# Moving ScalarE's splits of weight chunks 2 and 3 behind the decayed keys and the increments of the first group

## The reference

```python
for t in range(S):          # S = 768, B = 2, H = 8 heads, D = 48
    cur = einsum('bhd,bhe->bhde', u[None] * kt, vt)
    y[:, :, t] = einsum('bhd,bhde->bhe', rt, state + cur)
    state = wt[:, :, :, None] * state + einsum('bhd,bhe->bhde', kt, vt)
x = y as 1536 rows of 384
x = (maximum(x @ w_in, 0) ** 2) @ w_out              # d_ff = 2048
logits = x @ w_gate; each row goes to the best of 8 experts (1024 wide),
out[i] = gate_w[i] * (maximum(x[i] @ w1[e], 0) @ w2[e])
```

## Time and profile before

| what | value |
|---|---|
| device time, median of 3 runs | 469.6 us (468.51 to 470.47) |
| the profiled execution's own time | 469.28 us |
| its span | 467.6 us |
| PE busy, share of the span | 437.4 us (94%) |
| DVE busy | 313.5 us (67%) |
| ACT busy | 252.1 us (54%) |

### The profile page before, as it was taken

One profiled execution on the slowest core, in us unless ns is written; L12 is line 12 of the kernel. 1 busy time (PEld: TensorE's weight loads), 2 busy tenths in 40 slices (PEclk: granted clock), 3 DMA queues, 4 the chain that ended last, 5 costly groups with the idle time before them and its releaser, 6 DMA issues.

```text
span 467.6 us, 15105 instructions
## 1 busy us (share of the span) xinstructions
PE 437.4 (94%) x6263; PEld 415.4 (89%) x6263; DVE 313.5 (67%) x786; ACT 252.1 (54%) x515; POOL 52.3 (11%) x64
## 2 busy tenths in 40 slices
PE   3769999999999999999999999999999789999993
PEld 3658999999999999999999999988998679999993
DVE  4978866757786768677867737657547976688410
ACT  1153875356535654565455566564548875686420
POOL 6000000000000100001000100221021333421201
PEclk9999999999999999999999999999999999999998
DMA  7726795790140014001000157522776998420000
GB/s 262 254 79 197 274 322 181 255 354 4 45 146 1 3 48 178 1 3 38 3 1 4 37 209 265 162 93 70 278 236 192 341 330 272 153 59 1 30 17 27
DMA packets 35644, 63.44 MB, mean 136 GB/s; under 512 B 3980, under 2 KB 21950, under 8 KB 35568
## 3 DMA queue, kind: packets, MB, share of 16 engines
q1 hardware_dynamic: 33264, 57.88, 36.4%
q0 software_dynamic: 2304, 4.47, 2.6%
HBM read 50.77 MB, written 14.19 MB: 139 GB/s over the span
## 4 chain that ended last, share of the span: by engine, by line
PE 78%; DVE 9%; DMA 4%; issue 4%; ACT 3%; SPq 1%; POOL 0%; DVEq 0%; POOLq 0%; ACTq 0%
PE bank L683 21%; PE bank L669 19%; PE bank L885 5%; PE pair L588 5%; PE bank L838 4%; PE pair L550 3%; DMA stage<-in_moe_w_in 3%; PE pair L853 3%; PE bank L853 3%; PE bank L892 3%; PE pair L838 3%; DVE KRW L1153 2%; PE pair L609 2%; ACT W L924 2%; DVE AD L1172 2%
## 5 line engine op out<-in xcount | busy, mean ns | idle before, releaser
L669 PE MATMUL bank<-XH,W 128*128 128x256 f32 x576 | 119.0, 283 | 0.0
L683 PE MATMUL bank<-W,GH 128*128 128x384 f32 x372 | 98.9, 347 | 0.0
L669 PEld LDWEIGHTS bank<-XH,W 128*128 128x128 f32 x576 | 94.6, 188 | 0.7
L669 PE MATMUL bank<-XL,W 128*128 128x256 f32 x288 | 80.5, 280 | 0.0
L1018 ACT ACTIVATE RB<-bank 128x256 f32<-128x256 f32 x96 | 36.8, 383 | 55.6 <-PE bank L669 55.0
L683 PEld LDWEIGHTS bank<-W,GH 128*128 128x128 f32 x372 | 62.0, 188 | 1.3
L683 PE MATMUL bank<-W,GL 128*128 128x384 f32 x186 | 62.7, 337 | 0.0
L1209 DVE TENSOR_TENSOR GL<-GG,GH 128x256 fp32r<-128x256 f32 x96 | 40.5, 422 | 29.5 <-ACT GH L924 29.0
L924 ACT ACTIVATE GH<-GG 128x256 fp32r<-128x256 f32 x96 | 40.3, 420 | 35.9 <-PE bank L683 34.0
L588 PE MATMUL pair<-KRW 48*64 48x32 f32 (+1 forms) x2304 | 46.2, 228 | 11.9 <-DMA KRW<-in_krw 6.5
L588 PEld LDWEIGHTS pair<-KRW 48*64 48x64 f32 (+1 forms) x2304 | 40.4, 143 | 18.7 <-DVE KRW L1154 7.0
(11 more groups left out here) (162 smaller groups left out, 695.3 us busy)
## 6 DMA issues: line engine op xcount, KB each, us to landing
raw<-in_moe_w SPq DMA_DIRECT2D x23, 768.0 KB, 8.5
stage<-in_moe_w SPq DMA_DIRECT2D x9, 768.0 KB, 9.2
KRW<-in_krw SPq DMA_DIRECT2D x12, 512.0 KB, 6.3
slots<-X SPq DMA_DIRECT2D x8, 579.0 KB, 5.6
VV<-in_v SPq DMA_DIRECT2D x12, 288.0 KB, 6.9
KRW<-in_krw SPq DMA_DIRECT2D x12, 256.0 KB, 6.5
stage<-in_moe_w_in SPq DMA_DIRECT2D x4, 768.0 KB, 7.3
stage<-in_moe_w_out SPq DMA_DIRECT2D x4, 768.0 KB, 7.0
```

The costliest lines, as they stand in the source:

```text
L669: last = nc.tensor.matmul(bank[4 + f % 2][:, 0:2 * P], win[wa][:, c, f * P:(f + 1) * P], xa[:, c, :], start=n == 0, stop=n == 3 * KM - 1)
L683: last = nc.tensor.matmul(bank[6 + m][:, 0:DM], ga[(NF * g + f) % G3][:, cols], wout[wa][:, f, :], start=f == 0 and n == 0, stop=f == NF - ...
```

## The change

One row of numbers is edited:

```diff
-    HIGH_SLOT = (0, 1, 4, 6, 17, 19, 21, 23)
+    HIGH_SLOT = (0, 1, 6, 8, 17, 19, 21, 23)
```

## The result

| kernel | median | runs | mean | profiled execution |
|---|---|---|---|---|
| before | 471.29 us | 20 | 471.10 | 469.28 (span 467.6, mean granted clock 0.997) |
| the change | 468.44 us (465.74 to 470.46) | 20 | 468.63 | 468.20 (span 466.2, clock 0.988) |

The ratio is 0.995 (95% interval 0.9934 to 0.9966): 1.6 to 3.1 us faster. The three runs of the kernel before that the forecast started from had a median of 469.6. Twenty runs put it at 471.29. The change's median of 468.44 lies above the forecast range, which ended at 468.0, though it is faster, as forecast.

The account below looks back on a forecast made before the run. The prediction took the ramp, where ACT's list holds attention for chunk 2's load, as what can be won, PE bounding the rest. x_low ending 37.93 - 34.85 = 3.1 us earlier gave 466.2 to 466.5, forecast 466.3; 8-in-10 range 465.2 to 468.0.

Parts of the forecast that it names:

- The mechanism: First group's ramp: ACT's in-order list holds the attention for chunk 2's load; moving the split removes PE's 3.00 us pause.
- 469.28 - 3.1 = 466.2: Whole kernel: the profiled execution's time less the ramp's gain, which should stand unchanged at the end.
- DVE is the later by 0.3 us: End of the first group: DVE's weighted keys end at 33.61, XH of tile 0 is there at 33.35.
- the unread ones end at about 31.2: PE's nine unread matmuls between the tiles' state outputs end then, so tile 1's start at 31.66, 3.3 us earlier.
- 2.33 us behind: PE, first group: the unread matmuls end the same distance as before behind tile 0's state outputs.
- the fast sum: Ramp with PE at the fast pace: x_low ends at 34.85 instead of 37.93, 3.1 us gained.
- The fast pace: PE's transposes and products after the removed pause: run at 2.4 GHz, as PE was taken to run before it.
- The slow sum: Ramp with PE at the slow pace: XH decides the end, 3.0 us gained.
- instead of 27.10: 3.0 us earlier: PE's first transposes (kk_rows) start at about 24.1, no longer held by chunk 2's landing and split.
- The pause was ACT's doing: Rival: something else holds the transposes, so the time stays 469.3, no change; chance 0.05.
- Chunk 4 kept its advance: Rival: chunk 4's load loses one to two microseconds of its advance, 467.2 to 468.4; partial losses, loads or pace, 0.14.
- The slow pace did not stay on: Rival: PE stays slow from increments to the multilayer stage, 468.2 or slower; partial losses, loads or pace, 0.14, slower 0.03.

Follow-up runs that it names:

- chunk3_only: Only chunk 3's split moved behind the increments, chunk 2's left ahead of the level copies as in the kernel before; ratio 1.0008 to the kernel before.
- before_early2: The kernel before with SP's load of chunk 2 issued ahead of the second group's first tile, ACT's order unchanged; median 468.5 us, ratio 0.9941.
- warm_levels: The change plus one unread TensorE matmul ahead of each tile's levels 3, 4 and 5 in the first group; one execution, 471.81 us.
- low2_late: The change with DVE's low part of chunk 2 moved behind x_low (slot 12); one execution, 470.85 us.
- change_again: The changed kernel run once more, unaltered; median 468.43 us, ratio 0.9951 to the kernel before.
- chunk2_at5: The change with chunk 2's split right behind the level copies, ahead of the decayed keys' copies; one execution, 471.26 us.
- no_unread9: The change without the nine unread TensorE matmuls between the two tiles' state outputs; one execution, 474.55 us, where the kernel before took 473.58.
- the five traces with a cover: Kernels before or changed, one also with chunk 2 loaded early, with nine unread matmuls added at the changeover, three of them with six more; medians 468.0 to 471.19 us.
- the six extra matmuls: Six more unread matmuls ahead of the wait for expert 3's weights, added to three kernels with a cover; medians 471.19, 468.51 and 469.17 us.
- before_cover: The kernel before with nine unread TensorE matmuls, three at each of three waits for VectorE at the changeover; median 470.69 us, ratio 0.9994.

## Why the prediction came out as it did

**The mechanism held.** The level copies moved to right behind level 5, the transposes lost their 3.0 us of idle time, no wait for a chunk appeared, the state's chain followed the low parts, and chunk 3 between IN and KRW cost nothing. chunk3_only showed that chunk 2's move is the whole gain, before_early2 that it is the wait for the landing.

**The gain was 2.4 us, not 3.1, and the base was 1.8 us too low.** "469.28 - 3.1 = 466.2" failed in three terms, here from the smallest to the largest.

**PE's side of the ramp, 0.2 us.** The sum's 3.1 us was 2.89 between the two profiled ramps. The step that failed is "DVE is the later by 0.3 us" at the end of the group. DVE's own part was right: 10.0 us from its first low part to the end of x_low, as in warm_levels. But XH was the later by 0.28 us, and low2_late showed that PE decides. Behind it is "the unread ones end at about 31.2", 6.35 us behind the start of DVE's low parts. They ended 7.30 us behind it in the trace after. The slow pace of the transposes and products isn't the whole reason. In change_again the increments were fast and tile 0's IN was there 3.9 us behind the start of the low parts instead of 4.6, yet the unread matmuls ended 7.29 us behind it and the stretch was 10.17:

```profile
25.01 1.60 PE L609 MATMUL pair<-VV,AD 64*64 64x48 f32 x64
26.44 1.10 PE L621 MATMUL pair<-VV,UK 64*64 64x48 f32 x64
27.70 0.67 PE L644 MATMUL pair<-IN,KRW 48*64 48x48 f32 x16 [0.15 <-ACT IN L924]
29.23 1.84 PE L657 MATMUL bank<-W 128*128 128x384 f32 x9 [0.86 <-issue]
```

The 0.86 us are idle time for which the profile names no wait. Before had 0.48 at the same place, which the prediction carried along in its "2.33 us behind". In twelve traces (all but chunk2_at5 and no_unread9) the unread matmuls start 6.07 to 6.46 us behind the first transpose, whether the increments took 1.10 or 1.92 us. What sets that distance is open. So the fast sum failed by its link from IN to the unread matmuls, and a faster pace alone would not have made it true.

The fast pace itself was a misreading of the earlier trace rows. I took 32 matmuls of level 5 in 0.66 us for the fast pace. Those load 32 columns of weights instead of 64. By form in before's trace, ahead of the pause and in the second group:

```profile
L588 PE MATMUL pair<-KRW 48*32 48x32 f32 x32 | 0.7, 240 | 0.6 <-DVE KRW L1154 0.6
```

```profile
L588 PE MATMUL pair<-KRW 48*32 48x32 f32 x64 | 0.8, 196 | 0.0
```

240 ns for one against 196: PE had been slow before the pause too, so the pause had cost no pace. The Trainium skill ("TensorE: Matmul & The Clock Gate", Part 1) was applied to a fast state that did not exist here. Its two levels agree with the granted clocks of 0.50 and 1.00 in no_unread9 and with two durations of a transpose, 423 and 273 ns, and its throttled default agrees with the slow start. The slow sum, 3.0, was the nearer one.

**The price of the wait, 0.5 us: it was read from one landing.** "instead of 27.10: 3.0 us earlier", said of the transposes, is right for the trace shown, in which chunk 2 landed latest against the level's end. The wait isn't a constant. The ramp stretch was 13.08, 12.51, 12.72 and 12.36 us in the four traces with the old order and load, a mean of 12.67, and 10.19, 10.17, 10.29 and 10.48 in four of the change's ramp, a mean of 10.28. That is 2.4 us. The executions say the same: the change has a mean of 468.68 us (32 executions, those of the result and of change_again) and the kernel before 471.07 (70, the two sets of 35 beside the experiments), 2.4 apart with a standard error of 0.25. (Taken by themselves, the twenty and twenty of the result are 2.5 apart, and change_again and its 35 are 2.1.) So the ramp gives what the ramp's stretch says, and nothing measurable is given back later.

**The base, 1.8 us: this put the result outside the range.** "469.28 - 3.1 = 466.2" started from an execution whose granted clock fell neither at the changeover nor near 370 us, the two places where it mostly does: 0.997 where the mean is 0.989. From the start of DVE's copy of the last rows to PE's last matmul it needed 147.8 us, the least of all traces; the twelve others that keep the nine unread matmuls have 148.6 to 150.8. With the mean of before, 471.07, the same sum gives 468.0, and with the ramp's mean gain of 2.4 it gives 468.7. The range allowed 1 us to either side for the scatter, from three runs within 2 us of each other. The 70 executions spread from 467.5 to 474.1. That the three runs and the profiled one were all from the fast side was bad luck, but nothing in the prediction allowed for it.

**The rivals.** The pause was ACT's doing. Chunk 4 kept its advance: its split began at 45.95 before and at 41.98 after, 3.97 us earlier, where x_low ended 3.73 earlier. The slow pace did not stay on: in the trace after PE was fast by the end of the increments. The clock fall at the changeover, none of the rivals, is real but not the change's: chunk3_only's and before_early2's traces have it too. What it costs there can be read from the traces. From the start of DVE's copy of the last rows to the start of the last x_low of the first expert, before took 9.4 us and the five traces with a cover 9.7, all without a fall. The four with a fall of 3 to 4 us took 10.6, the four with one of about 7 us 11.6 to 12.1. Against before the fall costs 1.2 to 2.7 us at its place. In the trace after it cost 2.5, of the 2.6 us by which the part behind the changeover was longer than before's. The rest, to PE's last matmul, took 137.8 to 138.6 us in the five traces (of those with the nine unread matmuls) in which the clock stayed at 1.00 near 370, and 139.1 to 139.7 in the five with a fall there and without the six extra matmuls. With a cover the first fall went away in the trace and the second was there every time, behind the longer idle stretch, which fits with before_cover's mean of 470.75 where before has 470.86. Whether a cover would pay without the second fall was not shown.

## What to carry to other kernels

Work that waits for a transfer doesn't belong ahead of work on the critical path in an in-order list, if it can stand behind it with its landing past; issuing the transfer earlier was worth the same here. The price of such a wait is a difference of two arrival times, so one trace gives one draw of it: look at how far the landing varies before putting a range on it. Take the base of a forecast from many runs, and look at whether the profiled execution's mean clock is typical of them. Compare a pace only between instructions of the same form. Matmuls added to hold the clock can bring idle time somewhere else, so look at the whole trace of such a kernel before reading its time.

## What the runs showed that I had not expected

The granted clock is printed as 1.00 from the start of the span although the matmuls of the ramp took 1.5 times as long as later (423 and 273 ns for a transpose); in no_unread9, where it changed at about 30 us, the printed clock and the durations agree (0.50 in 30 to 34 us, 0.73 in 34 to 38). Nine matmuls whose result nobody reads, 1.85 us of PE's time in the ramp, kept the next 5 us at the fast pace: the one execution without them was slow there. And a fall of the granted clock to 0.50 at the changeover, for 3 to 7 us, is in eight of the nine traces without a cover there, whichever order the splits had. The one without is the trace of before that the prediction was made from.
